# Attention stage: the third projection behind the sums, q's three turns in a row, other PSUM banks for turns of results

## The reference

```
def phi(x):                                   # x is q or k, scaled
    proj = einsum('bhsd,md->bhsm', x, omega)  # 64 -> 128 features
    sq = sum(x * x, -1, keepdims=True) / 2.0
    h = proj - sq
    h = h - max(h, -1, keepdims=True)
    return exp(h) / sqrt(m)
q_p, k_p = phi(q_s), phi(k_s)
kv  = einsum('bhsm,bhsd->bhmd', k_p, v)       # the sums
z   = sum(k_p, axis=2)
num = einsum('bhsm,bhmd->bhsd', q_p, kv)      # the output
den = einsum('bhsm,bhm->bhs', q_p, z)[..., None] + 1e-06
x   = num / den                               # goes on to the dense layers
```

## Time and profile before

| | us |
|---|---|
| median of three runs | 771.92 |
| the profiled execution, its own time | 772.19 |
| its span, first to last instruction | 770.3 |
| start of sums(2), sums(14), sums(15) | 27.53, 124.07, 130.94 |
| TensorE busy, share of the span | 98% |

### The profile page before, as it was taken

One profiled execution on the slowest core, in us unless ns is written; L12 is line 12 of the kernel. 1 busy time (PEld: TensorE's weight loads), 2 busy tenths in 40 slices (PEclk: granted clock), 3 DMA queues, 4 the chain that ended last, 5 costly groups with the idle time before them and its releaser, 6 DMA issues.

```text
span 770.3 us, 15060 instructions
## 1 busy us (share of the span) xinstructions
PE 756.3 (98%) x5326; PEld 675.5 (88%) x5327; DVE 346.0 (45%) x892; ACT 314.3 (41%) x685; POOL 346.2 (45%) x288
## 2 busy tenths in 40 slices
PE   8999999999999999999999999999999999999996
PEld 7888888888888888888888888998999999999996
DVE  6887878211124435243334346783862331332231
ACT  4888888433242223322243222445324325325220
POOL 6898992344223222222232222258727627528421
PEclk9999999999999999999999999999999999999998
DMA  9888871020040000200020000460172613521121
GB/s 339 297 281 278 287 275 56 29 54 28 1 191 28 1 1 1 109 0 0 0 81 29 1 1 0 143 217 29 32 260 88 213 53 117 172 61 31 31 62 33
DMA packets 26602, 75.30 MB, mean 98 GB/s; under 512 B 3248, under 2 KB 4656, under 8 KB 26432
## 3 DMA queue, kind: packets, MB, share of 16 engines
q1 hardware_dynamic: 22864, 64.13, 23.5%
q0 software_dynamic: 3264, 10.03, 4.3%
q10 hardware_dynamic: 432, 0.59, 0.2%
HBM read 61.11 MB, written 13.63 MB: 97 GB/s over the span
## 4 chain that ended last, share of the span: by engine, by line
PE 85%; DVE 5%; POOL 3%; issue 2%; DMA 2%; ACT 1%; POOLq 0%; SPq 0%; DVEq 0%; ACTq 0%
PE pj L823 26%; PE nm L1035 14%; PE pj L1492 8%; PE tr L1035 6%; PE kv L1035 6%; PE kv L1536 6%; PE nm L1536 6%; PE nm L1492 5%; DMA qk<-in_qk_n 2%; PE pj L311 2%; PE kv L327 1%; DVE pj L580 1%; PE pj L1549 1%; PE nm L389 1%; POOL sqt L231 1%
## 5 line engine op out<-in xcount | busy, mean ns | idle before, releaser
L1008 POOL TENSOR_TENSOR gl<-sg,gh 128x512 fp32r<-128x512 f32 (+1 forms) x80 | 94.9, 1186 | 286.7 <-ACT gh L845 286.7
L839 DVE TENSOR_TENSOR sg<-pj,sg 128x512 f32<-128x512 f32 (+1 forms) x80 | 50.9, 637 | 211.5 <-ACT sg L832 211.4
L832 ACT ACTIVATE sg<-pj 128x512 f32<-128x512 f32 (+1 forms) x80 | 44.2, 553 | 140.2 <-PE pj L823 140.0
L823 PE MATMUL pj<-xh,win_h 128*128 128x512 f32 x256 | 100.0, 391 | 0.0
L823 PE MATMUL pj<-xh,win_l 128*128 128x512 f32 x256 | 99.6, 389 | 0.0
L823 PE MATMUL pj<-xl,win_h 128*128 128x512 f32 x256 | 99.6, 389 | 0.0
L845 ACT ACTIVATE gh<-sg 128x512 fp32r<-128x512 f32 (+1 forms) x80 | 47.2, 590 | 100.1 <-PE tr L1035 61.1
L969 DVE SCALAR_TENSOR_TENSOR raw<-pj,xT 128x512 f32<-128x512 f32 x96 | 62.5, 689 | 20.0 <-ACT pj L910 13.2
L1492 PE MATMUL pj<-xTh,W 128*128 128x288 f32 x320 | 71.3, 300 | 0.2 <-DVE xTl L1751 0.2
L1296 POOL TENSOR_TENSOR W<-wraw,W 128x1024 fp32r<-128x1024 f32 x28 | 66.3, 2399 | 8.2 <-ACT W L1292 8.2
L823 PEld LDWEIGHTS pj<-xh,win_l 128*128 128x128 f32 x256 | 48.1, 188 | 10.1
(11 more groups left out here) (303 smaller groups left out, 1788.1 us busy)
## 6 DMA issues: line engine op xcount, KB each, us to landing
wraw<-in_moe_w SPq DMA_DIRECT2D x7, 2048.0 KB, 10.5
ve<-in_v_z SPq DMA_DIRECT2D x16, 585.0 KB, 4.1
qk<-in_qk_n SPq DMA_DIRECT2D x14, 576.0 KB, 5.8
qkT<-in_qk_t SPq DMA_DIRECT2D x14, 576.0 KB, 6.3
y_rows<-ys SPq DMA_DIRECT2D x18, 256.0 KB, 2.4
stage<-in_moe_w_in SPq DMA_DIRECT2D x8, 512.0 KB, 6.9
y_early<-ys SPq DMA_DIRECT2D x16, 256.0 KB, 3.0
stage<-in_moe_w_out SPq DMA_DIRECT2D x4, 512.0 KB, 5.1
```

The lines of the kernel that those rows point to most:

```text
L823: mm = eng.matmul(ph[f % 3][:, 0:tiles_of(n) * P], w[f // F1A][:, c, f % F1A, :], x[:, c, :], start=(c == 0 and w is win_h and x is bh), s ...
L832: eng.activation(sg[f % 2][:, at], ph[f % 3][:, at], ACT.Sigmoid, scale=1.702).then_inc(a_sg, 1)
L839: eng.tensor_tensor(sg[f % 2][:, at], ph[f % 3][:, at], sg[f % 2][:, at], ALU.mult).then_inc(v_g, 1)
L1008: eng.tensor_tensor(gl[f % 3][:, at], sg[f % 2][:, at], gh[f % 3][:, at].bitcast(F32), ALU.subtract).then_inc(g_gl, 1)
```

## The change

On TensorE, in every step but 0 and 15, p2 moves from behind q's turn 1 to directly behind the sums. q's three turns then stand in a row, and after them the three turns of results. In step 0 the turns stand together ahead of p2. q's third turn goes to bank `kv` (it waited for a free `tr`; now it waits for `copy_kv`), and the turns of results go to `tr`, `nm[1]`, `kv` instead of `kv`, `nm[1]`, `kv`. The waits that guard the banks follow.

On ScalarE the three copies of q's turns stand in a row, and in even steps the first two copies of results stand behind them; b1 comes only then. In odd steps b1 comes behind the third copy.

```
@@ attention
+    qf_banks = (tr, nm[0], kv)
+    x_banks = (tr, nm[1], kv)
@@ sums
-            need(eng, a_kv, i)
             if a == 1 and not (isinstance(i, int) and i == 1):
                 need(eng, a_xs, 3 * n)
+            else:
+                need(eng, a_qf, 3 * i)
@@ turn_qf
             else:
-                eng.wait_ge(a_qf, 3 * i + 1)
-            bank = nm[0] if g == 1 else tr
+                eng.wait_ge(a_kv, i + 1)
+            bank = qf_banks[g]
@@ turn_x
             if g == 0:
                 eng.wait_ge(v_nm, 2 * OG * (n + 1))
-                eng.wait_ge(a_kv, unit + 1)
+                eng.wait_ge(a_qf, 3 * unit + 1)
             elif g == 2:
-                eng.wait_ge(a_xs, 3 * n + 1)
+                eng.wait_ge(a_qf, 3 * unit + 3)
@@ tensor, step
-            turn_qf(i, n, a, 0)
-            turn_qf(i, n, a, 1)
-            project(*x, 2)
+            else:
+                project(*x, 2)
+            for g in range(3):
+                turn_qf(i, n, a, g)
+            if isinstance(i, int) and i == 0:
+                project(*x, 2)
             if before:
-                turn_x(n - 1, 0, i)
-            turn_qf(i, n, a, 2)
-            if before:
-                turn_x(n - 1, 1, i)
-                turn_x(n - 1, 2, i)
+                for g in range(3):
+                    turn_x(n - 1, g, i)
@@ scalar, step
-            copy_qf(i, n, a, 0)
-            copy_qf(i, n, a, 1)
-            exps_b(*x, 1)
+            for g in range(3):
+                copy_qf(i, n, a, g)
             if before:
                 copy_x(n - 1, 0)
-            copy_qf(i, n, a, 2)
-            if before:
                 copy_x(n - 1, 1)
+                exps_b(*x, 1)
                 copy_x(n - 1, 2)
             else:
+                exps_b(*x, 1)
                 exps_a(*x, 0)
```

More of the change, by code:

```diff
@@ L354, in turn_x @@
                 eng.wait_ge(v_nm, 2 * OG * (n + 1))
-                eng.wait_ge(a_kv, unit + 1)
+                eng.wait_ge(a_qf, 3 * unit + 1)
             elif g == 2:
-                eng.wait_ge(a_xs, 3 * n + 1)
+                eng.wait_ge(a_qf, 3 * unit + 3)
             for j in range(3):
-                mm = eng.transpose((nm[1] if g == 1 else kv)[:, j * P:(j + 1) * P],
+                mm = eng.transpose(x_banks[g][:, j * P:(j + 1) * P],
                                    xs[:, 3 * g + j, :, :].rearrange("p h d -> p (h d)"), ident[:, :])
@@ L447, in copy_x @@
         def copy_x(n, g, bank=None):
-            bank = bank if bank is not None else nm[1] if g == 1 else kv
+            bank = bank if bank is not None else x_banks[g]
             eng.wait_ge(t_xs, 3 * n + g + 1)
```

## The result

The changed kernel takes 777.87 us, median of 6 runs (777.55 to 777.92), against 772.22 for the kernel before on the same chip (6 runs). The ratio is 1.0075 [1.0062, 1.0088]. It is slower, as forecast, but by 5.65 us instead of 3.3. The time lies 0.03 us inside the prediction's whole range (772.2 to 777.9) and above the forecast's own (773.7 to 776.8). That 777.6 is near 777.87 is luck.

What follows compares the result with a forecast made beforehand. The prediction took TensorE, busy for 98% of the span, as the bound. Pairs +1.0, step 1 +0.5 and step 14 +1.75 sum to +3.25, forecast 775.2 us; own range 773.7 to 776.8, whole range 772.2 to 777.9.

Steps and rivals of the forecast that it cites:

- That 777.6: Total time in us forecast by rival C, in which late squares add 2.4 us; chance 14%.
- p2 and the copies of q's turns: Even steps: p2 waits for b0, starts at 2.20 after the sums; q's first copy starts at 3.64 to 3.66, 1.02 later.
- ScalarE's chain in even steps: Up to a1: 1.02 later minus a gap of 0.32 makes 0.70 us; a1 ends at 8.42 instead of 7.72.
- its sums(13) can start at 8.52: End of even step 12: sums follow a1 by 0.10, so the step takes 8.52 instead of 8.28 us, +0.24.
- odd steps: TensorE idles 0.5 us ahead of the output, p1 stands about 0.1 for b2: 7.70 against 7.57, +0.13.
- The pairs together: sums(2) to sums(14): six pairs of 16.22 us plus 0.2 left for squares, 97.5 against 96.54, +1.0.
- the 1.44 us of late squares: Time lost in the old pairs beyond six times 15.85 us, via loads and GpSimd's squares; would absorb part of the cost.
- Step 1: First copy 0.92 us later and a third copy ahead of b1; sums(2) at 28.0 instead of 27.53: +0.5, between 0 and 0.7.
- Step 14: p2 waits for b0, q's copy comes 1.53 us later and all reaches sums(15): +1.75, between +1.4 and +1.9.
- A: Rival, faster: stalls for copies, 2.0 us, vanish and step 14 costs nothing if b1 starts early: 769.9 us; chance 10%.
- B: Rival, no change: loads and GpSimd set the pace, pairs and step 1 cost nothing, only step 14: 773.4 us; chance 18%.
- C: Rival, much slower: weights' casts end later, GpSimd's squares fall behind 0.4 us per pair, 2.4 more: 777.6; chance 14%.

Runs made afterwards that it cites:

- b: Changed kernel with ScalarE's copy of the third piece of results moved behind b2 in even steps 2 to 12: 777.25 us, ratio 1.0068.
- bf: Kernel b with a0 also moved behind b2 on ScalarE in odd steps: 775.19 us, ratio 1.0045.
- e8: Changed kernel with GpSimd's order altered to one `low` behind each unit's squares instead of two behind every second: 778.01 us, ratio 1.0080.
- c: Changed kernel with p2 put behind q's three turns in step 14 alone: 777.28 us, ratio 1.0075.
- d: Kernel before with only p2 moved directly behind the sums (not in step 0), banks and ScalarE's order as before: 781.74 us, ratio 1.0129.
- a2: Changed kernel with p2 behind q's three turns and b1 directly behind their copies, ahead of all copies of results: 771.34 us, ratio 0.9996.
- e5: Kernel a2 with GpSimd's order altered to one `low` behind each unit's squares instead of two behind every second: 769.65 us, ratio 0.9971.
- e9: Kernel e5 with p2 moved between q's turns 1 and 2 (its second and third): 774.98 us, ratio 1.0039.
- a: Changed kernel with p2 put behind q's three turns in every step, the rest of the change kept: 774.08 us, ratio 1.0033.

## Why the prediction was right in its direction and too small

**p2 and the copies of q's turns.** The time is right, nearly to the hundredth. The turn was to go out at 3.06 and the copy to follow at 3.64 to 3.66 from the sums; in step 12 they came at 3.08 and 3.67 (114.92 and 115.51 less 111.84), in step 2 the copy came at 3.66. The reason given for p2's start is right in step 14 alone. The prediction had p2 wait for b0 until 2.20. In step 12 b0 ended at 1.66 (112.61 + 0.89 less 111.84) and p2 started at 2.21 (114.05) without idle time, directly behind the sums, and so in every step from 1 to 13. The sums' own end and b0's forecast end lay within 0.1 us of each other, so the number came out right by luck. What the first copy waits for is the length of p2, not b0.

**ScalarE's chain in even steps.** Right too: a1 was to end at 8.42. a0 starts at 119.33, and with the 0.94 for two of the earlier trace rows a1 ends at 8.43.

**The step that failed is the one on p1,** "its sums(13) can start at 8.52". I had written that TensorE "stands for b2" ahead of p1 and never gave that wait a time. b2 ends at 7.66 in step 12 (118.58 + 0.92), p1 starts 0.15 later, at 7.81, and takes 0.86 to the sums: 8.67. The limit was max(a1, b2 + p1), and the second is later. In odd steps I did price b2 (end near 7.0, in fact 6.88 in step 3) and added "about 0.1" to the old sum; p1 at 7.02 and 0.87 behind it give 7.89. That is the same omission: 1.60 for p0 and p1 from the earlier trace rows is the time of an unbroken pair, and once p1 stands, only its own whole length counts from there. The earlier trace rows had that length, 0.86, and I used it for p2. b2 of step 12 can be read in the timeline of ScalarE before:

```profile
114.25 0.90 ACT L480 ACTIVATE feat<-pj,nb 128x128 f32<-128x128 f32 x3
```

It ended at 6.93 from the sums. With the forecast's own 0.70 of delay, 0.10 and 0.86 the even step is 8.59, and with b2 at 7.0 the odd one is 7.96: a pair of 16.55 instead of 16.22. Steps 12 and 13 took 8.67 + 7.89 = 16.56. Kernels b and bf are the test: with b2 early the even steps lose 0.15 and most odd ones 0.4.

**The pairs together.** Forecast +1.0, measured +3.8 (96.54 to 100.33). Steps 2 to 7 are 16.66 a pair rather than 16.56, and the even steps 8 and 10 take 9.03 and 9.00, which I did not foresee. The idea that part of the cost would fall into the 1.44 us of late squares holds: VectorE waits for them nowhere in the pairs, and in e8 the other order on GpSimd gains nothing there. Of the 2.8 that the forecast lacks (97.5 to 100.33), the two missed waits of p1 are 2.0, six times 16.56 less 16.22. Steps 8 and 10 together are 0.7 beyond the 8.67 of step 12, and steps 2, 4 and 6 another 0.3. The 0.2 that I had set aside for the squares was not needed.

**Step 1.** Forecast +0.5, between 0 and 0.7; measured +0.74 (7.15 to 7.89), just outside, since p1 stands for b2 here too. sums(2) started at 28.07, forecast 28.0, because sums(1) came 0.20 earlier.

**Step 14.** Forecast +1.75, measured +1.53. The copy began 4.26 behind the sums (forecast 4.21), and b0 was the cause of p2's wait. My account of it as a cost of p2's place alone was too simple: c shows that moving p2 back gives only 0.58, as b1 then meets the next copy that is not ready. In d, p2 first alone adds 1.38. Either edit alone brings most of the loss, and only both undone remove it but for 0.17 (a2).

**The sum.** 0.74 + 3.79 + 1.53 is 6.06, less the 0.20 by which sums(1) was earlier: 5.86 at sums(15) (130.94 to 136.80). The rest of the program was 0.36 shorter, which gives the 5.5 of the spans and fits the 5.65 of the medians.

**The rivals.** A asked whether b1 can pass a copy that is not ready; step 12 shows that it does not. B fell with the pairs: they did not stretch inside time that the loads set. C fell with the changed kernel's own waits, none of which is for squares in the pairs, and with e8. Its sign for it, longer waits of GpSimd for casts, was seen (1.8 to 2.7 us) and cost nothing.

Not settled: why steps 8 and 10, in the second loop, take 0.25 more than the other even ones. ScalarE stands 0.29 and 0.27 us ahead of their first copy of results. The kernel before has it too, with 0.15 (8.43 and 8.41 against 8.28 in step 12), e5 with 0.2, and d and e9 not at all. No kernel was made for it. Open too is why the even steps 2, 4 and 6 take 0.1 more than step 12.

## What to carry to other kernels

Where engines work in order, a product moved forward delays the products behind it, and on the engine that reads those everything queued behind their copies: here one projection of 0.87 us held up exponentials that had been ready for up to 2.4 us. Price a step as the latest of all its ends, and for an end that passes a wait, add the full length of what comes behind the wait, not its share of an unbroken row. Change the order on the producer and on the reader together (a and a2, e5 and e9), and expect a gain only where the chain that it shortens ends last (e5 and e8).

## What the runs showed that I had not expected

- The same edit on GpSimd is worth 1.56 us in the pairs of a2, 1.10 in those of before, and nothing in the changed kernel.
- Two edits of one change pull against each other: p2 first alone adds 9.8 us by sums(15) (130.94 to 140.76), the whole change 5.86.
- Moving one projection by one turn of 0.45 us (e5 to e9) costs 5.3 us.
- A projection of 12 that starts after a wait takes 0.87 to the sums (43.86 to 44.73). Ahead of a wait p0 still takes its length, so a pair with a wait of 0.2 between lasts 2.04 (42.69 to 44.73) against 1.60 for the unbroken pair of the earlier trace rows.
- From the end of b2 to the p1 that waits for it pass 0.14 to 0.15 us (43.72 to 43.86, 119.50 to 119.65), where I had taken 0.10.
